# A fused attention and two-layer mixing kernel: the head of the attention phase reordered, one product with w_k moved into the last pair of chunks, and for chunks 8 and 9 the output products ahead of the products with the state

## What is computed

```python
# linear attention with decay lam per head, in blocks b of 64 tokens
intra = (q_b @ k_b.T * Dmask) @ v_b          # Dmask[i, j] = lam ** (i - j) for i >= j
inter = (q_b * lam ** (pos + 1)) @ kv_state
out[b] = intra + inter
kv_state = lam ** 64 * kv_state + (k_b * lam ** (63 - pos)).T @ v_b

# channel mixing, x_prev is x shifted by one token
xk = mu_k * x + (1 - mu_k) * x_prev;  xr = mu_r * x + (1 - mu_r) * x_prev
x2 = sigmoid(xr @ w_r) * (relu(xk @ w_k) ** 2 @ w_v)      # w_k is 512 x 1024

# gated convolution, 5 taps over the tokens
out = (sigmoid(conv(x2, conv_w)) * (x2 @ w_val)) @ w_out
```

## Time and profile before

| what | us |
|---|---|
| median of 3 runs (lowest, highest) | 277.77 (277.58, 279.51) |
| the profiled execution | 278.59 |
| its span, first to last instruction | 276.5 |
| PE busy | 268.1 (97%) |
| DVE busy | 167.3 (60%) |
| ACT busy | 125.3 (45%) |
| POOL busy | 48.7 (18%) |
| granted TensorE clock | 1.00 of full speed |

### The profile page before, as it was taken

How to read it: one execution, slowest core, us unless ns; L and a number is a source line. 1 busy time by engine, 2 the same in 40 slices (tenths; PEclk the granted TensorE clock), 3 DMA queues, 4 the chain that set the end, 5 groups by cost and what they waited for, 6 DMA issues and landing times.

```text
span 276.5 us, 4258 instructions
## 1 busy us (share of the span) xinstructions
PE 268.1 (97%) x1740; PEld 225.0 (81%) x1740; DVE 167.3 (60%) x248; ACT 125.3 (45%) x223; POOL 48.7 (18%) x35
## 2 busy tenths in 40 slices
PE   8599988999999999999999999999999999999996
PEld 7589977888888888888888888888888888888885
DVE  4956981899979113455886535337978599425000
ACT  2137668769477213457821143749217305412121
POOL 1677757916900000000000000000000000000000
PEclk9999999999999999999999999999999999999999
DMA  7999995000000000000000000350000000310323
GB/s 253 414 405 409 406 406 229 0 0 2 0 0 0 2 0 0 0 0 2 0 0 0 5 0 0 117 188 0 0 0 2 0 0 0 116 38 0 114 78 114
DMA packets 7506, 22.83 MB, mean 83 GB/s; under 512 B 960, under 2 KB 1216, under 8 KB 7488
## 3 DMA queue, kind: packets, MB, share of 16 engines
q1 hardware_dynamic: 7344, 22.55, 21.1%
q10 hardware_dynamic: 144, 0.02, 0.0%
HBM read 19.42 MB, written 3.15 MB: 82 GB/s over the span
## 4 chain that ended last, share of the span: by engine, by line
PE 94%; DVE 2%; issue 1%; ACT 0%
PE ps L696 28%; PE ps L695 28%; PE ps L697 28%; PE ps L763 4%; PE ps L711 3%; PE ps L750 2%; PE ps L728 1%; DVE qdec L598 1%; DVE pT L505 0%; DVE state L522 0%; ACT out_sb L411 0%; DVE state L519 0%; DVE om L600 0%
## 5 line engine op out<-in xcount | busy, mean ns | idle before, releaser
L695 PE MATMUL ps<-xk_h,wk_h 128*128 128x512 f32 x96 | 37.5, 390 | 0.0
L697 PE MATMUL ps<-xk_h,wk_l 128*128 128x512 f32 x96 | 37.4, 389 | 0.0
L695 PE MATMUL ps<-kk_h,wv_h 128*128 128x512 f32 x96 | 37.3, 389 | 0.0
L696 PE MATMUL ps<-kk_l,wv_h 128*128 128x512 f32 x96 | 37.3, 389 | 0.0
L697 PE MATMUL ps<-kk_h,wv_l 128*128 128x512 f32 x96 | 37.3, 389 | 0.0
L696 PE MATMUL ps<-xk_l,wk_h 128*128 128x512 f32 x96 | 37.3, 389 | 0.0
L568 DVE SCALAR_TENSOR_TENSOR gate<-x,prm,gate 128x512 f32<-128x512 f32 x48 | 32.6, 744 | 0.0
L544 DVE SCALAR_TENSOR_TENSOR kk_f<-ps,ring 128x512 f32<-128x512 f32 x24 | 16.5, 688 | 23.8 <-ACT ring L364 23.8
L381 ACT ACTIVATE gate<-x,prm 128x512 f32<-128x512 f32 x12 | 8.6, 724 | 38.9 <-DVE x L554 38.9
L364 ACT ACTIVATE ring<-ps 128x512 f32<-128x512 f32 x24 | 14.3, 596 | 26.0 <-PE ps L697 26.0
L549 DVE TENSOR_TENSOR kk_l<-kk_f,kk_h 128x512 fp32r<-128x512 f32 x24 | 21.2, 883 | 1.8 <-ACT kk_h L368 1.8
(11 more groups left out here) (72 smaller groups left out, 498.0 us busy)
## 6 DMA issues: line engine op xcount, KB each, us to landing
qk<-in_qk SPq DMA_DIRECT2D x12, 512.0 KB, 11.2
kv<-in_kv SPq DMA_DIRECT2D x10, 512.0 KB, 12.0
out<-out_sb SPq DMA_DIRECT2D x11, 256.0 KB, 2.0
wk_raw<-in_w_k SPq DMA_DIRECT2D x4, 512.0 KB, 12.8
wv_raw<-in_w_v SPq DMA_DIRECT2D x4, 512.0 KB, 11.0
wr_raw<-in_w_r SPq DMA_DIRECT2D x2, 512.0 KB, 14.9
w_raw<-in_w_val SPq DMA_DIRECT2D x2, 512.0 KB, 4.4
w_raw<-in_w_out SPq DMA_DIRECT2D x2, 512.0 KB, 6.8
```

Source lines behind the costliest of these rows:

```text
L695: nc.tensor.matmul(to, left(0), right(0), start=(i == 0), stop=False)
L696: nc.tensor.matmul(to, left(0), right(1), start=False, stop=False)
L697: done = nc.tensor.matmul(to, left(1), right(0), start=False, stop=(i == last))
```

## The change

- SP's queue loads prm first (before: ACT's queue), then qk 0, qk 1, kv 0, qk 2, kv 1, qk 3, kv 2, kv 3.
- DVE makes qdec ahead of weigh(0); POOL runs decay_q(1) ahead of decay_k(1); PE runs inter(1) and attend(1) ahead of update(1).
- For the pair p = 4 (chunks 8 and 9, `OUT_FIRST`) PE runs attend ahead of inter; attend(8) opens the sum and waits for the banks (x_ready), inter closes it, and evacuate_x(4) also waits for inter.
- In the last pair PE runs hidden(0, 0) between inter(11) and attend(10). For it ACT makes w_k's high piece 0 right behind evacuate_x(3), and POOL its low piece behind its last decay_q. DVE makes the lows of pieces 1 and 2 (semaphore `wk_lo_mid`), POOL that of piece 3.
- value(0, 0) waits for w_v's lows piece by piece (before: for all four ahead of its first matmul).
- The last output chunk is cut at column 384 (before: 256), for product, copy and store.

```diff
--- before.py
+++ after.py
@@ -32,6 +32,8 @@
 OUT_CH = NT * CT
+CUTS = (0, 384, DM)
+OUT_FIRST = 4
 
...
@@ -145,7 +147,7 @@
             sem(z) for z in "wk_hi wk_lo wr_hi wr_lo wv_hi wv_lo w2_hi w2_lo".split()]
-        wk_lo_first = sem("wk_lo_first")
+        wk_lo_mid = sem("wk_lo_mid")
         (xk_part, xk_full, xk_hi, xk_lo, xr_part, xr_full, xr_hi, xr_lo) = [
...
@@ -179,6 +181,8 @@
 
+            if n // 2 == OUT_FIRST:
+                return not of_state and n % 2 == 0
             if not has_inter(n):
...
@@ -222,11 +226,16 @@
 
+            sp.dma_start(prm[:, :], prm_in).then_inc(prm_here, 16)
             load_qk(0)
...
             load_kv(0)
+            load_qk(2)
             load_kv(1)
-            for p in range(1, NP - 1):
+            load_qk(3)
+            load_kv(2)
+            load_kv(3)
+            for p in range(2, NP - 1):
                 load_qk(2 * p)
...
@@ -257,7 +266,7 @@
                     for half in range(2):
-                        cols = slice(half * DM // 2, (half + 1) * DM // 2)
+                        cols = slice(CUTS[half], CUTS[half + 1])
                         sp.wait_ge(out_ready, n + 1 + half)
...
@@ -297,9 +306,9 @@
             decay_k(0)
-            decay_k(1)
             pool.wait_ge(qdec_ok, PAIRS)
             decay_q(1)
+            decay_k(1)
             decay_q(2)
...
@@ -309,7 +318,7 @@
                 decay_q(2 * p + 1)
-            for i in range(1, 4):
+            for i in (0, 3):
                 low(wk, wk_raw, i, wk_hi, wk_lo)
...
@@ -324,6 +333,8 @@
                 act.wait_ge(att_done, 2 * p + 2)
+                if p == OUT_FIRST:
+                    act.wait_ge(inter_done, inters(2 * p + 1))
                 nc.scalar.copy(x[:, :, cols].rearrange("p (g a) i -> p g a i", g=2),
...
@@ -406,12 +417,11 @@
                     for half in range(2):
-                        cols = slice(half * DM // 2, (half + 1) * DM // 2)
+                        cols = slice(CUTS[half], CUTS[half + 1])
                         act.wait_ge(proj_done, n + 1 + half)
                         nc.scalar.copy(out_sb[t][:, c, cols],
-                                       ps[:, (bank_of("proj", t, c) + half) % 8, 0:DM // 2]).then_inc(out_ready, 1)
-
-            act.dma_start(prm[:, :], prm_in).then_inc(prm_here, 16)
+                                       ps[:, (bank_of("proj", t, c) + half) % 8, 0:CUTS[half + 1] - CUTS[half]]).then_inc(out_ready, 1)
+
...
@@ -429,11 +439,12 @@
             evacuate_x(3)
+            high(wk, wk_raw, 0, wk_here, wk_hi)
             fade(9)
...
             evacuate_x(4)
-            for i in range(3):
+            for i in range(1, 3):
                 high(wk, wk_raw, i, wk_here, wk_hi)
...
@@ -592,11 +603,11 @@
             dve.wait_ge(dec_ok, H)
-            weigh(0)
             dve.wait_ge(zero_ok, 1)
...
                                              zeros[:, :], 1.0, ALU.mult, ALU.add).then_inc(qdec_ok, 1)
+            weigh(0)
             nc.vector.tensor_scalar(om[:, :], prm[:, MU:MU + 2 * KT], -1.0, 1.0, ALU.mult, ALU.add).then_inc(om_ok, 1)
...
@@ -628,7 +639,8 @@
                 if p == 5:
-                    low(wk, wk_raw, 0, wk_hi, wk_lo_first)
+                    low(wk, wk_raw, 1, wk_hi, wk_lo_mid)
+                    low(wk, wk_raw, 2, wk_hi, wk_lo_mid)
             for k in range(KT):
...
@@ -689,9 +701,11 @@
         def _(pe):
-            def three_pass(to, pairs):
+            def three_pass(to, pairs, ahead=None):
                 last = len(pairs) - 1
                 for i, (left, right) in enumerate(pairs):
+                    if ahead:
+                        ahead(i)
                     nc.tensor.matmul(to, left(0), right(0), start=(i == 0), stop=False)
...
@@ -749,7 +763,8 @@
                                                 qd[rows_of(row), n % 4, a * P:(a + 1) * P],
-                                                start=(opens(n, True) and a % 2 == 0), stop=False, skip_group_check=True)
+                                                start=(opens(n, True) and a % 2 == 0),
+                                                stop=(n == 2 * OUT_FIRST + 1 and a % 2 == 1), skip_group_check=True)
                 last.then_inc(inter_done, 1)
...
@@ -757,13 +772,16 @@
                 pe.wait_ge(p_ready, 2 * n + 2)
+                if n == 2 * OUT_FIRST:
+                    pe.wait_ge(x_ready, OUT_FIRST)
                 for a in range(PAIRS):
...
                                                 start=(opens(n, False) and a % 2 == 0),
-                                                stop=(a % 2 == 1 and n % 2 == 1), skip_group_check=True)
+                                                stop=(a % 2 == 1 and n % 2 == 1 and n // 2 != OUT_FIRST),
+                                                skip_group_check=True)
                 last.then_inc(att_done, 1)
...
@@ -775,10 +793,10 @@
                         pe.wait_ge(p_ready, 2 * NCH)
-                if t == 0 and n == 0:
-                    pe.wait_ge(wk_lo_first, 1)
-                elif t == 0 and n % 2 == 0:
-                    pe.wait_ge(wk_lo, n // 2)
+                if t == 0 and n in (0, 6):
+                    pe.wait_ge(wk_lo, n // 6 + 1)
+                if t == 0 and n in (2, 4):
+                    pe.wait_ge(wk_lo_mid, n // 2)
                 if t == 0 and n == 2:
...
@@ -805,11 +823,15 @@
                     pe.wait_ge(kk_lo, FT * (t + 1))
-                    pe.wait_ge(wv_lo, 4)
+
+                def piece_of_wv(f):
+                    if t == 0 and m == 0 and f % 2 == 0:
+                        pe.wait_ge(wv_lo, f // 2 + 1)
+
...
                            [(lambda z, f=f: wv[z][:, f * DM + m * P:f * DM + (m + 1) * P], lambda z, f=f: kk[z][:, f, :])
-                            for f in range(FT)]).then_inc(v_done, 1)
+                            for f in range(FT)], piece_of_wv).then_inc(v_done, 1)
 
...
@@ -840,7 +862,7 @@
                 if CT * t + c == OUT_CH - 1:
-                    halves = [(bank, 0, DM // 2), ((bank + 1) % 8, DM // 2, DM)]
+                    halves = [((bank + i) % 8, CUTS[i], CUTS[i + 1]) for i in range(2)]
                     pe.wait_ge(out_ready, CT + 1)
...
@@ -856,9 +878,9 @@
             scores(2)
-            update(1)
             inter(1)
             attend(1)
+            update(1)
             scores(3)
...
@@ -873,15 +895,21 @@
                     scores(2 * p + 3)
+                if p == OUT_FIRST:
+                    attend(2 * p)
+                    attend(2 * p + 1)
                 inter(2 * p)
                 inter(2 * p + 1)
-                attend(2 * p)
-                attend(2 * p + 1)
+                if p + 1 == NP:
+                    hidden(0, 0)
+                if p != OUT_FIRST:
+                    attend(2 * p)
+                    attend(2 * p + 1)
                 if p + 1 < NP:
...
             for t in range(NT):
-                for n in range(FT):
+                for n in range(1 if t == 0 else 0, FT):
                     hidden(t, n)
...
```

## The result

The kernel after takes 280.37 us (median of 6 runs, 280.12 to 281.08), the kernel before 278.38 beside it (6 runs): ratio 1.0075, 95% interval 1.0049 to 1.0100. So it is slower, by about 2.0 us, where 0.4 us faster was forecast; 280.37 lies outside the range of 276.1 to 279.3. The profiled execution took 280.23, its span is 278.4. In all that follows a profile is one execution and can lie beside its kernel's median, by 0.2 us for the kernel before (278.59) and by up to 0.9 us elsewhere (e11, 278.88 against 277.99).

The account below looks back on a forecast made before the run. PE, with 94% of the chain, was taken to bound the kernel: its dense stretch's start and density, and the tail. 0.2 us at the value product plus 0.2 in the tail made 0.4: 277.77 becomes 277.4, range 276.1 to 279.3.

Parts of the forecast that it names:

- prm, the loads and the head: Kernel's start: prm lands at 2.5, first inter at 11.2 instead of 13.04; PE enters later pairs about 1.0 us earlier.
- hidden(0,0) between inter(11) and attend(10): Last pair: hidden(0,0) starts at 41.45 behind POOL's low, attend(11) ends at 46.2, PE is 1.6 us ahead at the next hidden.
- What is queued behind attend(11): ACT, DVE and POOL up to the value product: evacuate_x(5) at 46.25, kk_low(0,7) ends at 77.5, PE waits 1.4, 0.2 us gained.
- C's collision: Follow-ups' theory, not a prediction rival: POOL's low of piece 0 and DVE's mix_low collide, with new_state(10) queued behind.
- The cut at 384: Tail, last output chunk: 128-column matmuls 0.067 us each, 0.2 us gained; bounds 0.2 gained to 1.6 lost.
- Chunks 8 and 9: Attend before inter there: same matmuls in another order, zero either way, from minus to plus 0.69 us.
- The pause at 43.75: PE's second "issue" pause, 0.80 us: should shrink or go, with twelve long matmuls (2.7 us) now ahead of it.
- B: Rival at the tail: twelve narrow matmuls at the warm-up's pace, 0.213 us each, 1.75 us more, 279.1; chance 0.22.

Follow-up runs that it names:

- e11: Kernel before with only attend ahead of inter for chunks 8 and 9: 277.99 us, ratio 0.9977.
- e5: Kernel after with POOL's low of w_k's piece 0 waiting until DVE has done all four mix_low of xk: 279.89 us, ratio 1.0056.
- e12: Kernel before with hidden(0, 0) between inter(11) and attend(10), w_k's high piece 0 behind evacuate_x(3), its low left on DVE: 279.43 us, ratio 1.0030.
- e1: Kernel after with the last chunk cut at 256 again: 279.91 us, ratio 1.0068.
- e7: Kernel before with only the cut at 384: 278.70 us, ratio 1.0018.
- e9: Kernel after with the cut at 256, e5's wait, and ACT's high copies of w_k piece 3 and w_r ahead of evacuate_x(5): 278.09 us, ratio 0.9993.
- e3: Kernel after with DVE's mix_low(0,3) behind new_state(10) instead of ahead of it: 279.23 us, ratio 1.0026.
- e10: Kernel before with the change's head alone, as e4, but prm issued by ACT again: 281.57 us, ratio 1.0086.
- e4: Kernel before with the change's head alone (prm first on SP, load order, new order of qdec, decay_q(1), inter(1) and attend(1)): 278.46 us, ratio 0.9999.
- e6: Kernel after with mix_low(0,3) behind new_state(10), hidden(0, 0) behind attend(11) and the cut at 256: 277.85 us, ratio 0.9988.
- e8: Kernel after with e5's wait, hidden(0, 0) behind attend(11) and the cut at 256: 278.20 us, ratio 0.9988.
- e2: Kernel after with hidden(0, 0) put back behind attend(11): 278.75 us, ratio 1.0014.

## Why the prediction was wrong

- **prm, the loads and the head**: right in size. prm 1.7 us to landing, dec at 2.44, first inter at 10.91 (11.2 said), scores(4) held by qk 4 at 16.25 (16.6 said), kv 10 late by 0.2.
- **hidden(0,0) between inter(11) and attend(10)**: this step failed. It had inter(11) ending near 41.0 and hidden(0, 0) at 41.45, held by POOL's low alone. It did not ask what else runs while POOL's low runs: DVE's mix_low(0,3), with new_state(10) behind it. The rows to see it were there: the earlier trace rows shows four mixes at 7.69 us beside POOL, and the next step of the prediction even used it ("take turns"). Measured: mix_low 2.84 instead of 0.68, inter(11) ending near 43.1, 2.1 us later than said, and hidden(0, 0) at 43.07, 1.6 later. POOL's low itself ended at 41.44, close to the 41.3 worked out. e5 removes just this and gets 0.9 us of it back at hidden(0, 0).
- **What is queued behind attend(11)**: the mechanism was right and its length too (11.5 us); its start, 46.25, was mis-sized by 1.8 us: 1.6 from the step above, 0.2 for the twelve matmuls and the attends. So kk_low(0,7) ended at 79.22 instead of 77.5, and PE paused as named. With the 31.22 us that the profiles show from evacuate_x(5) to value(0, 0), a start at 46.25 would have given 77.47, so the forecast of this step stood or fell with the step above. What was underrated is the risk in the margin: there are 0.8 us between kk_low and the value product, and once they are used up each microsecond by which attend(11) moves back counts in full, while PE's being ahead counts for nothing. e12 shows this without C's collision: 1.0 us lost.
- **The cut at 384**: the term was mis-sized. I took 0.067 us a matmul from the slope, with 0.120 as the next bound; measured 0.11. The tail loses 0.3 to 0.5 us (e1, e7) instead of gaining 0.2. The 81 ns of the Trainium skill (TensorE: Matmul & The Clock Gate, Back-to-back issue gap) are nearer, but below the 0.11 us measured here with float32r as well.
- **Chunks 8 and 9**: zero was said; alone it is 0.2% faster (e11), for a reason that stays open.
- **The pause at 43.75**: gone, as said; in that place PE now waits for the state.
- **Rivals**: B had the right direction and, with 0.11 us a matmul, a small part of the size. None had DVE as the engine that makes PE wait at inter(11). A slower outcome through kk_low was within reach of the working and was not priced.

The sum of the two profiles: value(0, 0) 1.4 later and 0.15 for its weight load, 0.45 for the cut: 2.0 us, by which the last copy ends later (276.43 against 274.43). The medians differ by 2.0, the spans of these two executions by 1.9.

## What to carry to other kernels

When work is moved onto an engine that stretches another's work, as POOL and DVE do here, list what the other engine runs in that window and what stands behind it in its queue: a stretched small operation costs little itself, its successor may be what the critical engine needs. And before moving a product ahead of the last step of a phase, look at what that last step releases: the product gains its own length at most once, while every chain that starts behind the delayed step is late in full, and it decides as soon as its margin (here 0.8 us) is used up. Copies that depend on loads alone belong ahead of an evacuation that waits for PE, not behind it (e9: 1.3 us, if the gains of e1 and e5 add up).

## What the runs showed of the hardware that was not expected

- float32r matmuls with 128x128 weights and 128 columns stand 0.112 us apart, those with 256 columns 0.120 and with 384 columns 0.174 (512: 0.227): below 256 columns nearly nothing is saved.
- A DVE mix_low of 0.68 us that starts 0.5 us behind a POOL subtraction of 2.4 us takes 2.84 and ends 0.56 us behind POOL's end (42.00 and 41.44); in e3 it starts 0.6 us behind and takes 2.33, ending 0.55 behind (41.54 and 40.99). It does its work when POOL is through, instead of sharing. POOL's own takes 2.80 where it starts beside a mix_low that is already running, 2.36 in e5.
- In e10 2.35 us of waiting ahead of attend(0) were followed by a granted clock of 0.50 from 10 to 12 us; the kernel before waits 1.77 us there and keeps 1.00.
- The pause of the kind "issue" near 43.5 us, in the middle of the last attend, is there in the profiles of the kernel before, e4, e6, e7, e8 and e11, and not where hidden(0, 0) is run ahead of the attends (after, e1, e3, e5, e9, e12), nor in e2 and e10, where PE had just waited for the state. That fits instructions that arrive late unless PE is held up otherwise; it was not tested by itself.
